# Value products of a banded attention kernel, issued as four tiles of 32 queries instead of two of 64

## What is computed

```python
keep = (pos_k < n_global) | ((rel >= 0) & (rel < n_local))        # n_global 8, n_local 96
scores = q @ k.T / 8 - slope[h] * dist;  scores[~keep] = -1e9
a = softmax(scores);  attn = a @ v                                 # fp32
x = attn as (batch, 768, 512)
u = x + low_rank_mix(x);   x2 = u + relu(u @ w_ch1) @ w_ch2        # 512 -> 2048 -> 512
out = sigmoid(xr @ w_r) * (relu(xk @ w_k) ** 2 @ w_v)              # xk, xr: shifted blends of x2
```

## Time and profile before

| | |
|---|---|
| median of 3 executions | 544.78 us (544.54 to 545.2) |
| the profiled execution's own time | 544.91 us |
| its span, first to last instruction | 543.1 us |
| granted TensorE clock | 1.000 of full speed |
| instructions | 9465 |
| TensorE matmul busy | 528.7 us, 97% |

### The profile page before, as it was taken

One profiled execution on the slowest core, in us unless ns is written; L12 is line 12 of the kernel. 1 busy time (PEld: TensorE's weight loads), 2 busy tenths in 40 slices (PEclk: granted clock), 3 DMA queues, 4 the chain that ended last, 5 costly groups with the idle time before them and its releaser, 6 DMA issues.

```text
span 543.1 us, 9465 instructions
## 1 busy us (share of the span) xinstructions
PE 528.7 (97%) x3584; PEld 493.1 (91%) x3584; DVE 196.8 (36%) x529; ACT 133.5 (25%) x288; POOL 265.2 (49%) x282
## 2 busy tenths in 40 slices
PE   3999999999999999999999999999999999999997
PEld 2777787899999999999999999999998998998996
DVE  4867777412232223222122221222342342343223
ACT  2755566321111111111111101112321321321321
POOL 4589454329001700029910369830797798698000
PEclk9999999999999999999999999999999999999999
DMA  8743325002200310004420000000001001001001
GB/s 207 250 137 94 93 88 185 4 1 79 77 0 0 111 45 0 0 0 136 174 78 0 0 0 1 0 0 1 0 2 58 0 0 58 1 0 58 0 0 58
DMA packets 24602, 27.06 MB, mean 50 GB/s; under 512 B 14208, under 2 KB 14208, under 8 KB 24576
## 3 DMA queue, kind: packets, MB, share of 16 engines
q1 hardware_dynamic: 24288, 25.93, 15.0%
q10 hardware_dynamic: 288, 0.79, 0.5%
HBM read 23.57 MB, written 3.15 MB: 49 GB/s over the span
## 4 chain that ended last, share of the span: by engine, by line
PE 95%; POOL 2%; issue 1%; DMA 1%; DVE 0%; POOLq 0%; DVEq 0%
PE bank L497 25%; PE bank L509 24%; PE bank L553 12%; PE bank L562 12%; PE bank L577 6%; PE bank L364 4%; PE bank L397 4%; PE bank L372 4%; PE bank L404 2%; POOL w1l L1011 1%; PE bank L410 1%; DMA v_in<-in_v 1%; PE bank L412 1%; POOL w1h L1009 0%; DVE result L929 0%
## 5 line engine op out<-in xcount | busy, mean ns | idle before, releaser
L880 DVE SCALAR_TENSOR_TENSOR HL<-bank,HH 128x384 fp32r<-128x384 f32 x64 | 35.7, 558 | 173.6 <-ACT HH L684 173.6
L684 ACT ACTIVATE HH<-bank 128x384 fp32r<-128x384 f32 x64 | 31.5, 493 | 233.4 <-PE bank L497 233.4
L497 PE MATMUL bank<-UH,w1h 128*128 (+1 forms) x256 | 86.3, 337 | 0.0
L509 PE MATMUL bank<-HL,w2h 128*128 128x384 f32 x256 | 86.1, 336 | 0.0
L509 PE MATMUL bank<-HH,w2h 128*128 128x384 f32 x256 | 86.1, 336 | 0.0
L497 PE MATMUL bank<-UH,w1l 128*128 (+1 forms) x256 | 86.0, 336 | 0.0
L497 PE MATMUL bank<-UL,w1h 128*128 (+1 forms) x256 | 85.9, 335 | 0.0
L509 PE MATMUL bank<-HH,w2l 128*128 128x384 f32 x256 | 85.8, 335 | 0.0
L1009 POOL TENSOR_SCALAR w1h<-raw 128x2048 fp32r<-128x2048 f32 x5 | 9.6, 1912 | 126.3 <-PE bank L509 126.3
L607 ACT ACTIVATE probs<-probs,neg_max 128x256 f32<-128x256 f32 (+1 forms) x96 | 41.0, 481 | 30.2 <-DVE neg_max L765 30.2
L509 PEld LDWEIGHTS bank<-HL,w2h 128*128 128x128 f32 x256 | 48.1, 188 | 0.0
(11 more groups left out here) (108 smaller groups left out, 981.0 us busy)
## 6 DMA issues: line engine op xcount, KB each, us to landing
raw<-in_moe_w_ch SPq DMA_DIRECT2D x8, 1024.0 KB, 6.3
v_in<-in_v SPq DMA_DIRECT2D x8, 384.0 KB, 4.2
out<-result SPq DMA_DIRECT2D x12, 256.0 KB, 2.1
q_in<-in_q SPq DMA_DIRECT2D x7, 384.0 KB, 4.7
k_in<-in_k SPq DMA_DIRECT2D x7, 384.0 KB, 5.0
raw<-in_moe_w_v SPq DMA_DIRECT2D x2, 1024.0 KB, 5.4
raw<-in_moe_w_k SPq DMA_DIRECT2D x2, 1024.0 KB, 5.1
raw<-in_moe_w_r SPq DMA_DIRECT2D x1, 1024.0 KB, 5.2
```

Of the source, the lines that this page charges most:

```text
L497: mm = pe.matmul(bank[4 + f % 2][:, 0:BLK], w[:, kt, f * P:(f + 1) * P], x[:, kt, ds(blk * BLK, BLK)], start=kt == 0 and n == 0, stop=kt = ...
L509: mm = pe.matmul(bank[d][:, 0:BLK], w[:, f, d * P:(d + 1) * P], x[:, f % 2, :], start=f == 0 and n == 0, stop=f == FQ - 1 and n == 2)
L684: act.activation(HH[:, f % 2, :], bank[4 + f % 2][:, 0:BLK], ACT.Relu).then_inc(hid_high, 1)
L880: dve.scalar_tensor_tensor(out=HL[:, f % 2, :], in0=bank[4 + f % 2][:, 0:BLK], scalar=0.0, in1=HH[:, f % 2, :].bitcast(F32), op0=ALU.max, ...
```

## The change

The range of 128 queries at L396 is cut in steps of GLOB = 32 instead of at 64. Each product has 32 stationary columns and the same 66 moving columns, and writes to 32 PSUM partitions (0, 32, 64 or 96 on). The operands, the bank, the accumulation flags and the semaphores stay.

```diff
@@ -393,7 +393,7 @@
                                 src = v_in[:, p % 2, t, h, :]
                             else:
                                 src = v_in[:, p % 2, c - places[0], h, :]
-                            for r in (slice(0, P // 2), slice(P // 2, P)):
+                            for r in (slice(a, a + GLOB) for a in range(0, P, GLOB)):
                                 mm = pe.matmul(bank[O_BANK][r, (2 * i + h) * DV:(2 * i + h + 1) * DV],
                                                probs_t[:, n % 2, h, c * P + r.start:c * P + r.stop], src,
                                                start=c == places[0], stop=c == places[-1])
```

## The result

The changed kernel took 546.15 us in the median of 19 executions, the kernel before 544.91 in 19 beside them: ratio 1.0024, 95% interval 1.0015 to 1.0032, or 1.2 us more. The prediction had 544.5 us, no change.

A forecast was written before the change was run, and what follows sets the result against it. TensorE's matmuls were taken to bound the kernel, busy 528.7 of 543.1 us. The terms gave 544.91 - 0.65 + 0.34 = 544.6 us, forecast as 544.5 us, no visible change, with a range of 543.4 to 549.8 us.

The forecast's parts named there:

- step 1: Value product: twice the matmuls and loads, four tiles side by side, two passes of 58 ns a place as before; term 0.
- step 2: Start of each phase: first weight load of 32 columns instead of 64 is shorter; 24 x 0.027 = 0.65 us saved.
- step 3: End of each phase: last of four tiles starts 14 ns later; 24 x 0.014 = 0.34 us lost.
- step 4: Edges between tile shapes, about 0.15 us per phase: number of form changes stays, term 0, bound 1.2 us either way.
- Step 5: TensorE's instruction fetch: 1408 more instructions, covered by fetching ahead, term 0; uncovered, six packets would cost 6.6 us.
- A: Value product slower: only two tiles at a time, or 29 ns a matmul, 234 ns a place; 565.4 us, chance 0.17.
- the 25 ns: Skill's rule that matmul starts are never under about 25 ns apart: a place at least 200 ns, kernel 14.6 us slower.
- B: Value product slower: the start offset of four tiles is paid in each pass, 4.9 us more; 549.7 us, chance 0.08.
- C: Slower: instruction fetch not covered (551 us), or products not side by side (far above 565 us); chance 0.03.
- D: Faster: passes some 3 ns shorter or edges a third smaller, 542.5 us; or passes halved, 534.5 us; chance 0.07.

The follow-up runs named there:

- e8: e6 with each value product in one piece of 128 columns instead of two of 64; 555.58 us in a single execution, 10.7 us more than e6.
- e9: e5 (four tiles of 32) with 34 moving columns instead of 66 from the second unit on; 542.07 us in a single execution.
- e10: e6 (two tiles of 64) with 34 moving columns instead of 66 from the second unit on; 544.09 us in a single execution.
- e2: Kernel before with 123 more instructions in the general branch that is never taken; 550.28 us, ratio 1.0089.
- e5: Changed kernel with TensorE's two branches exchanged, so that no jump stands behind the attention; 546.81 us, ratio 1.0031.
- e7: Changed kernel with 191 never-executed TensorE instructions of the general branch left out; 544.53 us, ratio 0.9987.
- e1: Changed kernel with 41 never-executed instructions of the general branch left out (last copy of the mixing); 546.61 us, ratio 1.0028.
- e11: Kernel before with the same 191 unused instructions left out as in e7; 544.61 us, ratio 0.9992.
- e4: Changed kernel run once more with no edit, on another chip; 545.97 us, ratio 1.0017.
- e12: e7 once more, on the same chip as e11; 544.59 us, ratio 0.9988.
- e6: Kernel before with TensorE's two branches exchanged as in e5; 544.89 us, ratio 0.9997.

## Why the prediction was wrong, step by step

**Steps 1 to 4 held.** The pass stayed at 58 ns with four tiles side by side (step 1), and the larger of load and moving columns sets it (e8, e9, e10). The phase got shorter by 26 ns where 27 - 14 = 13 were forecast: the first load gave 26 to 30 ns (step 2), the later last tile took 11 of the 14 (step 3), and each place got about 1.5 ns shorter, some 10 ns a phase, which had no term. The edge of a phase (step 4) did not change beyond that; e8 gives it a size, about 0.30 us.

**Step 5 failed.** It gave the fetch of instructions a term of 0 because none of it is a stall "in the straight code from 50 to 97 us", and named six uncovered packets, 6.6 us, as the price if the cover were gone. The straight code from 50 to 97 us was the wrong place to look; it has no such stall in the changed kernel either. The attention ends with one jump, at 103.8 us, over the general branch; its 193 ns are a row of the trace before that was not read. That jump took 1.34 us longer where its landing block was on its way (the changed kernel) and 3.5 us longer where it had not been ordered (e2), and a fall of the clock came on top of the longer one; the price is neither 0 nor a packet's 1.1 us. On the profiled executions the sum closes: the attention ends 0.6 us earlier, L461 takes 1.34 us more, and the hidden layer starts, and the span ends, 0.8 us later. Beside this the fetch very likely cost the 0.2 us in the third phase, ahead of the stretch that step 5 had looked at.

**The rivals.** A (two at a time, or 29 ns each) and the 25 ns weighed with it are refuted by the changed kernel itself, 0.115 us for eight matmuls or 14 ns each, and by e9, 7.5 ns each. B had the direction (slower, by up to 4.9 us) and the wrong mechanism: no pass got longer. The range, 543.4 to 549.8 us, holds the measured 546.15 only by luck, since it reached that far up for B. C was the right family, at a chance of 0.03, and put at 551 us as a general shortage of fetching; its sign, a gap inside a phase of L397, shows once. Of D the trace has a part, a pass shorter by under 1 ns instead of 3, and no shorter edge; its 542.5 us is also a slip, as 544.78 - 0.65 - 1.1 - 1.2 is 541.8.

**Stays open:** where the borders of the blocks lie; why the load of v took 5.8 us in e5; what slowed the executions of e5 at full clock; whether the change of form makes all of a tiled phase's edge; and how the 1.24 us of the medians divide, since only the profiled executions show the jump (1312 and 1532 ns in two of them).

## To carry to other kernels

Before a change that alters how many instructions an engine runs, find the taken jumps on the path and what the engine has to do while each is fetched; read their rows as one reads waits. Unused code between a branch and what follows is not free: e2 lost 5.3 us by 123 instructions that never ran, and e7 took 191 away and got the whole loss back. It depends on where the jump lands: 41 fewer changed nothing in e1, nor did 191 fewer in the kernel before (e11). Of tiles, in the fp32 products of this case: the pass lasts as long as the longer of load and moving columns, so cutting the stationary side below the moving one brings nothing but a shorter first load.

## What the runs showed of the hardware that was not expected

- A held jump ended 2.5 to 2.8 us after a packet of code began, whether that packet had been ordered 1.0 us before the jump (changed kernel, e1; 1.3 in e4) or 1.0 us after it (e2, 3.7 us in all). A jump with a fetch under way that it did not need took 0.19 us (e7, e12).
- Behind the idle 3.1 us of e2 and 2.75 us of e5 TensorE's granted clock was at 0.50, 1.2 GHz; behind 1.3 us in the changed kernel it stayed at 1.00.
- The edges of a phase in column tiles cost some 0.30 us more than those of a phase in the whole array (e8 against e6, an estimate), some ten times what four tiles save against two (0.03 us a phase).
- Four column tiles take a load and a matmul each in 30 ns: eight of each in 60 ns (e9).
